# Chunked attention with memory keys before two expert stages: keys laid out in 40-column blocks, denominators from a column of ones beside V, K and Q loaded by thirds of a batch

## What the kernel must compute

```python
# attention: batch 4, 8 heads, 768 positions, head dimension 64, 8 memory keys
for c in range(24):                                   # chunks of 32 queries
    keys = positions 32c-16 .. 32c+40, cut at the ends of the sequence
    k_full = concat(mem_k, k[keys]);  v_full = concat(mem_v, v[keys])
    scores = scale * q_c @ k_full.T;  scores -= max(scores)
    a = exp(scores);  a = a / (sum(a) + 1e-9)
    out[c] = a @ v_full
x = out as [3072 tokens, 512]
x = ((x @ w_a) * (x @ w_b)) @ w_out                   # d_ff 1536
P = exp(x @ w_gate - max), then 8 rounds of row and column normalisation
out = sum over 8 experts of P[:, e] * (relu(x @ w1[e]) @ w2[e])     # F = 1024
```

## Time and profile before

| what | value |
|---|---|
| three timed runs | 2747.78, 2753.53, 2756.3 us |
| the profiled execution | 2742.24 us, of which span 2740.6 us |
| mean granted TensorE clock of it | 0.994 |
| PE busy | 2675.2 us (98%) |
| PE weight loads busy | 2213.7 us (81%) |
| DVE, ACT, POOL busy | 1390.5, 783.9, 513.9 us |
| L666 matmuls | 5550, 1396.9 us |
| L741 matmuls | 5472 in two forms, 1154.1 and 219.1 us |

### The profile page before, as it was taken

One profiled execution on the slowest core, in us unless ns is written; L12 is line 12 of the kernel. 1 busy time (PEld: TensorE's weight loads), 2 busy tenths in 40 slices (PEclk: granted clock), 3 DMA queues, 4 the chain that ended last, 5 costly groups with the idle time before them and its releaser, 6 DMA issues.

```text
span 2740.6 us, 37670 instructions
## 1 busy us (share of the span) xinstructions
PE 2675.2 (98%) x15648; PEld 2213.7 (81%) x15648; DVE 1390.5 (51%) x2047; ACT 783.9 (29%) x1277; POOL 513.9 (19%) x432
## 2 busy tenths in 40 slices
PE   7889999999999999999999999999999999999999
PEld 6767878878777888888888888888888888888887
DVE  2464554454568455455464554544546544545544
ACT  4544332232333333333332221222222212222211
POOL 0036520020254545545430000000001000000000
PEclk9989999999999999999999999999999999999999
DMA  7536543433355565555645334333333443343342
GB/s 184 141 91 242 219 186 149 159 145 139 146 173 173 193 208 175 202 201 174 208 156 196 130 129 167 127 138 158 127 148 147 158 158 138 127 169 127 131 165 88
DMA packets 133545, 437.94 MB, mean 160 GB/s; under 512 B 56320, under 2 KB 89088, under 8 KB 101888
## 3 DMA queue, kind: packets, MB, share of 16 engines
q1 hardware_dynamic: 133376, 435.54, 43.8%
HBM read 308.63 MB, written 126.88 MB: 159 GB/s over the span
## 4 chain that ended last, share of the span: by engine, by line
PE 92%; DVE 3%; ACT 2%; issue 1%; POOL 1%; DMA 0%; DVEq 0%; ACTq 0%; POOLq 0%
PE bank L666 44%; PE bank L741 43%; PE bank L582 2%; PE bank L607 1%; PE bank L630 1%; PE bank L601 1%; DVE tmp L1160 1%; PE bank L618 0%; ACT PT L866 0%; DVE Y L1193 0%; ACT QT L855 0%; DVE Y L1251 0%; POOL X L525 0%; DVE hid L1256 0%; DVE hid L1312 0%
## 5 line engine op out<-in xcount | busy, mean ns | idle before, releaser
L666 PE MATMUL bank<-X,W 128*128 128x512 f32 x5550 | 1396.9, 390 | 16.4 <-ACT tmp L960 4.9
L666 PEld LDWEIGHTS bank<-X,W 128*128 128x128 f32 x5550 | 1040.3, 188 | 242.0 <-issue 20.4
L741 PE MATMUL bank<-W,hid 128*128 128x512 f32 x4608 | 1154.1, 389 | 2.7 <-DVE Y L1190 2.7
L741 PEld LDWEIGHTS bank<-W,hid 128*128 128x128 f32 x4608 | 864.9, 188 | 182.6 <-DVE Y L1190 3.1
L1190 DVE SCALAR_TENSOR_TENSOR Y<-bank,gate,Y 128x512 f32<-128x512 f32 x720 | 539.6, 750 | 568.9 <-PE bank L741 561.2
L525 POOL TENSOR_TENSOR X<-Y,X 128x1024 fp32r<-128x1024 f32 x30 | 78.9, 2637 | 1095.8 <-ACT X L912 1095.8
L1018 ACT ACTIVATE hid<-tmp 128x512 fp32r<-128x512 f32 x192 | 121.4, 632 | 354.8 <-DVE tmp L1157 274.7
L741 PE MATMUL bank<-hid,W 128*128 128x512 f32 x864 | 219.1, 389 | 1.2 <-issue 1.2
L956 ACT ACTIVATE tmp<-bank 128x512 f32<-128x512 f32 x132 | 79.0, 599 | 486.5 <-PE bank L666 486.3
L1312 DVE SCALAR_TENSOR_TENSOR hid<-bank,hid 128x512 fp32r<-128x512 f32 x192 | 132.6, 691 | 162.5 <-ACT hid L1018 162.4
L741 PEld LDWEIGHTS bank<-hid,W 128*128 128x128 f32 x864 | 162.1, 188 | 35.3 <-issue 1.6
(11 more groups left out here) (85 smaller groups left out, 1102.5 us busy)
## 6 DMA issues: line engine op xcount, KB each, us to landing
W<-w_kept SPq DMA_DIRECT2D x88, 1792.0 KB, 8.6
w_kept<-W SPq DMA_DIRECT2D x44, 1792.0 KB, 6.7
W<-w_kept SPq DMA_DIRECT2D x76, 1024.0 KB, 4.8
w_kept<-W SPq DMA_DIRECT2D x38, 1024.0 KB, 4.9
raw<-in_moe_w_dram SPq DMA_DIRECT2D x64, 512.0 KB, 6.1
Vw<-in_v_dram SPq DMA_DIRECT2D x176, 56.0 KB
out_dram<-Y SPq DMA_DIRECT2D x24, 256.0 KB, 6.4
Kr<-in_k_dram SPq DMA_DIRECT2D x3, 1536.0 KB, 7.6
```

The source lines that it names most:

```text
L666: last = nc.tensor.matmul(into[:, :], W1[:, c % 2, ws, w_slot, kc, :], X[:, pos, xs, kc, :], start=(start and kc == 0 and n == 0), stop=(k ...
L741: last = nc.tensor.matmul(into[:, :], lhsT, rhs, start=(j == 0 and n == 0), stop=(j == 1 and n == 2))
```

## The change

Seven edits, all in attention:

1. `KT` is laid out in blocks of 40 columns: 32 keys and behind them the 8 memory keys. 64 neighbouring columns hold a chunk's 56 window keys and one copy of the memory's keys, so that `scores` is one product of 32 by 64 for each chunk and head. Line 607 is gone. ACT writes a K unit with two activations of half the size, and the memory's keys with one activation to all 24 blocks, one to the left pad and one to the right.
2. V is laid out in the same order of keys, so a chunk's 56 rows fall into two pieces (32 rows and 24 rows) with the memory's 8 values between them: three DMAs for each chunk and head parity, 24 for every quad.
3. `Vw` has six slots, one for each quad of a batch, and a 65th column of ones. `weigh_v` multiplies by 65 columns, so that the denominator comes out of it. `denominators` with its sum, its zeroing and its wait are gone. Absent keys have zero in `Vw`, ones included, set by POOL at the start; `sp.wait_ge(s_zero, 8)` holds the first V load until that is done.
4. `quotients` first adds the epsilon (two instructions from PSUM) and takes the reciprocal, then multiplies.
5. `PT` and `On` have one buffer where they had two.
6. K and Q are loaded by thirds of a batch (256 rows of each head, 512 KB), each third into its own part of `Kr` or `Qr`. A unit is 128 of these rows, every second one. Each quad waits only for the units that it needs.
7. The units are spread anew: 5 ahead of quad 0, then 2, 2, 2, 5, 2, 2 for quads 0 to 5, and 2 or 3 up to r = 13, then 4, 3, 4, 4; none from r = 18. A quad's first unit is done ahead of weigh_v.

```diff
             def load_v(r):
-                b, g, slot = r // G, r % G, r % 3
-                if r >= 3:
-                    sp.wait_ge(a_o, r - 2)
+                b, g = r // G, r % G
+                if b > 0:
+                    sp.wait_ge(a_o, r - G + 1)
                 for f in range(2):
                     for c in range(4):
...
-                        sp.dma_start(Vw[at:at + s1 - s0, slot, c],
-                                     v[b, f::2, s0:s1, :].rearrange("h s d -> s h d")).then_inc(s_v[slot], 16)
-                        if s0 > start:
...
-                        if s1 < start + WIN:
...
-                        if g < 3:
-                            at = 64 * f + WIN
-                            sp.dma_start(Vw[at:at + MEM, slot, c], mem).then_inc(s_v[slot], 16)
+                        sp.dma_start(Vw[at:64 * f + CHUNK, g, c, :, 0:HD],
+                                     v[b, f::2, s0:start + CHUNK, :].rearrange("h s d -> s h d")).then_inc(s_v[g], 16)
+                        at = 64 * f + BLK
+                        sp.dma_start(Vw[at:at + s1 - start - CHUNK, g, c, :, 0:HD],
+                                     v[b, f::2, start + CHUNK:s1, :].rearrange("h s d -> s h d")).then_inc(s_v[g], 16)
+                        at = 64 * f + CHUNK
+                        sp.dma_start(Vw[at:at + MEM, g, c, :, 0:HD],
+                                     mem_v[b, f::2].rearrange("h m d -> m h d")).then_inc(s_v[g], 16)
...
+            load_k(0, 0)
             load_mem(0)
+            load_q(0, 0)
+            load_k(0, 1)
+            sp.wait_ge(s_zero, 8)
             load_v(0)
+            load_q(0, 1)
+            load_k(0, 2)
             load_v(1)
+            load_q(0, 2)
             load_v(2)
             load_mem(1)
+            load_k(1, 0)
+            load_q(1, 0)
             load_v(3)
...
+            for r in range(G + 1, R):
+                b, g = r // G + 1, r % G
+                load_v(r)
+                if b < B and g == 1:
                     load_mem(b)
+                    load_k(b, 0)
+                if b < B and g == 2:
+                    load_q(b, 0)
...
                 for hp in range(HP):
                     for c in range(4):
                         for f in range(2):
-                            nc.tensor.matmul(b_s[f][32 * c:32 * c + 32, hp * KEYS:hp * KEYS + WIN],
-                                             qt[rows, hp, at:at + CHUNK], kt[rows, hp, at + PAD - LEFT:at + PAD - LEFT + WIN],
-                                             start=True, stop=True)
-                for hp in range(HP):
-                    for f in range(2):
-                        last = nc.tensor.matmul(b_s[f][:, hp * KEYS + WIN:(hp + 1) * KEYS],
-                                                qt[rows, hp, at:at + QUAD], kt[rows, hp, 0:MEM], start=True, stop=True)
+                            last = nc.tensor.matmul(b_s[f][32 * c:32 * c + 32, hp * KEYS:(hp + 1) * KEYS],
+                                                    qt[rows, hp, at:at + CHUNK], kt[rows, hp, col:col + KEYS],
+                                                    start=True, stop=True)
                 last.then_inc(a_s, 1)
 
             def transpose_p(r):
                 pe.wait_ge(a_exp, r + 1)
-                if edge(r):
-                    pe.wait_ge(a_pad, edges_to(r))
...
             def quotients(r):
                 dve.wait_ge(a_o, r + 1)
+                for f in range(2):
+                    nc.vector.tensor_scalar(rsum[:, f, :], b_o[f][:, 0:HP * (HD + 1)].rearrange(
+                        "p (j n) -> p j n", j=HP)[:, :, HD], EPS, None, ALU.add).then_inc(a_den, 1)
+                dve.wait_ge(a_den, 2 * r + 2)
+                nc.vector.reciprocal(rsum[:, :, :], rsum[:, :, :]).then_inc(a_rs, 1)
                 dve.wait_ge(a_rs, r + 1)
...
-            denominators(R - 1)
             quotients(R - 1)
```

More of the change, by code:

```diff
@@ L281, in first_use @@
             return BUILDS.index(w) if w in BUILDS else None
[L285 to L305, removed]
@@ L306, in build, with third @@
-        UNIT_ORDER = FIRST_UNITS + [u for us in QUAD_UNITS for u in us]
[L307 to L315, removed]
+        MK, KU, QU = range(3)
+        def third(b, kind, m):
+            return [(b, kind, m, 0), (b, kind, m, 1)]
+        FIRST_UNITS = [(0, MK, 0, 0), *third(0, KU, 0), *third(0, QU, 0)]
@@ new lines, in build @@
+        QUAD_UNITS = [third(0, KU, 1), third(0, QU, 1), third(0, KU, 2), third(0, QU, 2), [], []] + [[] for _ in range(R - G)]
+        for b in range(1, B - 1):
+            QUAD_UNITS[G * b - 3] += [(b, MK, 0, 0), *third(b, KU, 0)]
+            for i, (kind, m) in enumerate(((QU, 0), (KU, 1), (QU, 1), (KU, 2), (QU, 2))):
+                QUAD_UNITS[G * b - 2 + i] += third(b, kind, m)
+        LAST_UNITS = [(B - 1, MK, 0, 0)] + [u for m in range(TH) for kind in (KU, QU) for u in third(B - 1, kind, m)]
@@ new lines, in build, with units_to, units_for @@
+        for i, (n0, n1) in enumerate(((0, 2), (2, 5), (5, 9), (9, 13))):
+            QUAD_UNITS[R - G - 4 + i] += LAST_UNITS[n0:n1]
+        UNIT_ORDER = FIRST_UNITS + [u for us in QUAD_UNITS for u in us]
+        assert len(set(UNIT_ORDER)) == len(UNIT_ORDER) == B * UNITS and len(QUAD_UNITS) == R
+        def units_to(unit):
+            return UNIT_ORDER.index(unit) + 1
+        def units_for(r):
+            b, g = r // G, r % G
+            return units_to(((b, QU, 0, 1), (b, KU, 1, 1), (b, QU, 1, 1), (b, KU, 2, 1), (b, QU, 2, 1),
+                             (b, QU, 2, 1))[g])
@@ L645, in _ @@
                 nc.tensor.matmul(b_ot[:, 0:P], ident[:, :], ident[:, :], start=True, stop=True)
-            for b, i in FIRST_UNITS:
-                transposed(b, i)
+            for unit in FIRST_UNITS:
+                transposed(unit)
             for r in range(R):
@@ new lines, in unit_copy @@
+                    nc.scalar.activation(kt[:, :, 0:LEFT].rearrange("p h (b n) -> p h b n", n=MEM),
+                                         mem.unsqueeze(2).to_broadcast([P, HP, 2, MEM]), ACT.Copy)
+                    nc.scalar.activation(kt[:, :, KCOLS - RIGHT:KCOLS], mem, ACT.Copy).then_inc(a_tc, 1)
+                elif kind == KU:
+                    part = of[:, :].rearrange("p (h a g i) -> p h a g i", h=HP, a=8, g=2)
+                    for g in range(2):
+                        at = S // CHUNK // TH * BLK * m + LEFT + g * (LEFT + MEM) + j
+                        first = kt[:, :, at:at + 1]
+                        into = bass.AP(first.tensor, first.offset, [first.ap[0], first.ap[1], [BLK, 8], [2, 8]])
+                        last = nc.scalar.activation(into, part[:, :, :, g, :], ACT.Copy)
+                    last.then_inc(a_tc, 1)
+                else:
+                    nc.scalar.activation(qt[:, :, bass.ds(2 * P * m + j, P, 2)],
+                                         of[:, :].rearrange("p (h n) -> p h n", h=HP), ACT.Copy,
+                                         scale=SCALE).then_inc(a_tc, 1)
@@ L921, in _ @@
                 exps(r)
-                for b, i in QUAD_UNITS[r]:
-                    unit_copy(b, i)
+                for unit in QUAD_UNITS[r]:
+                    unit_copy(unit)
                 if r == G + 1:
```

216 lines of the change are left out of this document (99 added, 117 removed).

## The result

| | before | after |
|---|---|---|
| timed beside each other, medians | 2750.81 us (2747.78 to 2756.3) | 2818.59 us (2818.2 to 2819.98) |
| ratio | | 1.0245, 95% interval 1.0226 to 1.0265 |
| span of the profiled execution | 2740.6 us | 2816.5 us |
| mean granted TensorE clock | 0.994 | 0.976 |
| start of weigh_v(23) | 195.8 us | 269.4 us |

The kernel became 67.8 us slower, 75.9 in the two profiled spans. The forecast was 2805 and 51.6 us slower. Of the 75.9 us, 73.6 lie ahead of weigh_v(23). Behind it are 2.3 us, and there TensorE's granted clock was 0.50, half speed, in the first 6 us (269 to 275), where it was 1.00 in the kernel before (196.6 to 202 us).

A forecast was written before the change was run, and what follows sets the result against it. SP's issuing of V loads would bound attention: 3.5 + 12.3 + 224.6 + 4 + 2 = 246.4 us to weigh_v(23), 50.6 later, 51.6 with the clock; added to 2753.5 this gave 2805 us, range 2780 to 2835.

The forecast's parts named there:

- The mechanism: Attention: 576 V loads against 312, all on SP's queue, 9.4 us a quad where PE needs less than 5.
- The other issues between V loads: SP's queue: 21 thirds, three memory-key loads, two weight loads and the gate's, 12.3 us, none of them waiting.
- V issues with the clogging by thirds: SP's queue: 576 V loads at 0.39 us, 224.6 us, plus 4 us for slower issues behind K and Q loads.
- Landing: End of attention: the last V load's arrival ahead of weigh_v(23), 2 us taken, bounds 0 and 3.7.
- Slow clock behind weigh_v(23): Start of the expert stage: PE, idle in front of V, may start at half clock, 1 us, bounds 0 and 3.
- the V issue: SP's queue: each V load taken at 0.39 us, from 0.386 in the stretch from 147.26 to 159.57 us.
- SP clogged throughout: Rival, SP's queue: K and Q portions make 0.48 us a V load normal, +99 us, 2853; at 0.43 +71, 2824; chance 15%.
- The cost of thirds: SP's queue: V loads issued slower behind K and Q loads, 4 us taken, bounds 0 and 20.
- The faster rival: SP's queue: V issues hidden, PE stays the bound, weigh_v(23) at 162 us, 2720 us; chance 3%.
- TensorE's own gain of 34 us: Attention: without V loading, PE reaches weigh_v(23) some 34 us earlier (23 + 12 + some slow clock - 3).
- edge waits: Ahead of line 618, seven gaps of 1.7 us behind edge quads, waiting for DVE's zeroing, would go: 12 us.
- The signs: Trace of attention: V issues 0.39 us apart until 244 us, quads 9 to 10 us apart, low clock, weigh_v(23) near 246.

The follow-up runs named there:

- The three kernels with 32, 16 and 16 V loads a quad on SP: After with 32-row V loads cut in two, 2908.7 us; memory's loads issued by ScalarE, 2767.6; memory's values loaded once a batch and copied by GpSimd, 2764.5.
- the fastest version: After with V loads a quad split 8 SP, 4 ACT, 4 GpSimd, memory's values copied, K and Q thirds of the last two batches earlier: 2732.3 us.
- the run with that part alone: Before plus ones column, six V slots, single buffers, no zeroing, memory's values copied by GpSimd; line 607 kept: 2739.9 us, ratio to before 0.9978.

## Why the prediction was right, and where its terms were off

*The mechanism: right.* SP's issuing took the place of TensorE as the bound of attention. The three kernels with 32, 16 and 16 V loads a quad on SP move with it, and the kernel before without its V loads does not.

*The terms of the sum, forecast and measured.* First V load 3.5 us, measured 3.6. The other issues between V loads 12.3, measured 12.8 for 27 of them. V issues with the clogging by thirds 224.6 + 4 = 228.6, measured 251.3, from start to start. Landing 2, measured 1.7 from the start of the last issue. The sum of these is 246.4, measured 269.4. Slow clock behind weigh_v(23) 1, measured 2.3.

*The step that was mis-sized is the V issue: 0.39 us taken, 0.437 measured.* The medians of the three kinds (317, 391, 308 ns, and 0.043 us of gap) make 0.382, 220 us in all. The other 31 us are, to 24 us, what the 28 issues over 0.7 us take beyond that, 24 of them beside an instruction fetch; to 5 us the 23 issues between 0.45 and 0.7 us, most of which K and Q cause; and small pauses. The stretch of 32 loads from which the 0.386 came holds one issue over 0.7 us, the slower stretch from 112.89 us holds three, two of them beside a fetch, and I put the slower one down to Q. The trace of before could have shown it: 23 of its 28 V issues over 0.7 us overlap a fetch, and these 28 take 34.9 us.

*Where luck helped.* The cost that came, 0.437, lies above the 0.37 to 0.42 that the forecast claimed for itself. It fits the rival "SP clogged throughout" at its lower end (0.43, 71 us later, 2824), with other causes than that rival names. The range of 2780 to 2835 held 2818.6 because it took in the lower half of that rival. And the time flatters the sum: in the profiled spans the change is 75.9 us where 51.6 were forecast, 24.3 too few, while the timed difference was 67.8 and the median of before 2.7 us lower than the 2753.5 taken, which leaves 13.6.

*The cost of thirds: right.* 24 x 0.28 = 7 us by the run without K and Q, 4 were taken, bounds 0 and 20. That the thirds themselves would be late for TensorE, 25.7 us of waits, was not foreseen; the end did not hang on it.

*The faster rival: out.* No V issue of after took less than 273 ns, and the mean lies far above the 0.307 us that it needed. The prediction named the Trainium skill, "DMA: Bandwidth & Descriptors", section "Issuing engines are not separate DMA queues", by which the time to initiate a DMA "is usually small relative to the DMA itself". For loads of 8 KB here that rule misleads: moving 192 of them to another engine's queue, with the same transfers, gave 51 us.

*TensorE's own gain of 34 us: too large, as far as the runs can tell.* The quad was right (4.67 us), the total not: 12 us with V's loads left out behind batch 0, 12.8 in the fastest version (183.0 against 195.8). What was put at nothing became waits once the quads were shorter: idle stretches ahead of the score products, and the order of ACT's and DVE's operand work in the last quads. The 12 us of edge waits did go, but in the run with that part alone about as much came back elsewhere.

*The signs.* Most came: SP waits for no weigh_v, the clock of attention is low (0.77), lines 607 and the zeroing are gone, the tail is unchanged but for 2.3 us. Three did not come as told. The V issues are 0.437 us apart and end at 268, not 0.39 and 244. The quads are mostly 10 to 12 us apart, not 9 to 10, and not evenly: weigh_v(15) to (17) come 15 to 20 us behind the one before, (18) to (21) 3 to 8. Line 639 waits in most quads, but hardly in 15 to 19. The start of weigh_v(23), 269.4, lies just under the 270 from which the prediction would have blamed the thirds.

## What to carry to other kernels

Count the DMA instructions on each queue and multiply them by their issue time, before anything else of a new data layout: a layout that saves TensorE 1 us a quad in score products may cut each load in three, and a queue that was already busy for about 162 of 191 us, as SP's was before, is then the bound. In these profiles it does not show as busy time of any engine; it shows as "issue" gaps ahead of the consumer and as the queue's own back-to-back starts. When a queue is that full, the cure is to spread the loads over the other engines' queues, or to copy repeated data on an idle engine.

## What the runs showed of the hardware that was not expected

- The time SP needs to issue a load does not go by its own size alone: 0.30 to 0.33 us if it or the load ahead of it has 8 rows, 0.43 us for 16 rows behind 16 and for 32 rows behind 32 (64 and 128 pieces of 256 bytes). One pair of before, 8 rows behind 40, took 0.51 us.
- TensorE's instruction fetches hold up SP's DMA issuing: 25.2 us for 33 added fetches, 0.76 us each, and 24 of 28 long issues beside one. By what they block each other was not tried.
- TensorE too seems to wait for its fetches: with the score products four times 46 of its 52 idle stretches over 0.3 us end 2.1 to 3.0 us after a fetch began.
